# Linear attention and two expert layers on one core: routing in three rounds of 99 levels, GpSimd's order in the first expert, and one branch at the end

## The reference, cut to what matters

```python
state = alpha[:, :, t, :, None] * state + einsum(k[:, :, t], v[:, :, t])   # for each t
y[:, :, t] = einsum(q[:, :, t], state)
...
logits = x @ w_gate                       # 3072 x 8
for idx in np.argsort(-logits.flatten()): # greedy, the largest logit first
    tok, e = idx // E, idx % E
    if assigned[tok] >= 0 or counts[e] >= cap: continue
    assigned[tok] = e; counts[e] += 1
...
for e in range(E):
    out[assigned == e] = np.maximum(x[assigned == e] @ w1[e], 0.0) @ w2[e]
...
g = x @ w_gate2                           # x is the experts' output here
return (g / (1 + exp(-g)) * (x @ w_val)) @ w_out
```

## Time and profile before

| | |
|---|---|
| median of three runs | 913.92 us |
| the profiled execution | 914.68 us |
| its span in the profile | 912.9 us |
| PE busy | 853.5 us, 94% |
| VectorE busy | 512.2 us, 56% |
| ScalarE busy | 280.4 us, 31% |
| GpSimd busy | 253.2 us, 28% |
| mean granted TensorE clock | 0.966 |

### The profile page before, as it was taken

One profiled execution on the slowest core, in us unless ns is written; L12 is line 12 of the kernel. 1 busy time (PEld: TensorE's weight loads), 2 busy tenths in 40 slices (PEclk: granted clock), 3 DMA queues, 4 the chain that ended last, 5 costly groups with the idle time before them and its releaser, 6 DMA issues.

```text
span 912.9 us, 17432 instructions
## 1 busy us (share of the span) xinstructions
PE 853.5 (94%) x6582; PEld 801.4 (88%) x6582; DVE 512.2 (56%) x1057; ACT 280.4 (31%) x505; POOL 253.2 (28%) x200
## 2 busy tenths in 40 slices
PE   6999996699969999999999999999999999999991
PEld 4788874399869999999999999999999999999991
DVE  6999985637824464457445634664365536533330
ACT  1344441223214232422332332333233332333210
POOL 2322210165944023403240414050305130522001
PEclk8999997699979999999999999999999999999996
DMA  8789960400310022003200410030013002300000
GB/s 333 267 331 334 337 220 35 153 13 23 100 43 26 0 91 72 27 0 103 60 26 0 129 42 18 20 127 26 17 63 101 17 9 69 95 26 1 1 1 29
DMA packets 25858, 77.27 MB, mean 85 GB/s; under 512 B 3808, under 2 KB 10464, under 8 KB 22880
## 3 DMA queue, kind: packets, MB, share of 16 engines
q1 hardware_dynamic: 22752, 67.39, 21.2%
q0 software_dynamic: 3072, 9.44, 3.3%
HBM read 67.38 MB, written 9.44 MB: 84 GB/s over the span
## 4 chain that ended last, share of the span: by engine, by line
PE 74%; POOL 3%; DVE 2%; issue 1%; DMA 1%; ACT 0%; POOLq 0%; ACTq 0%
PE ps_up L1572 44%; PE ps_acc L1572 26%; PE ps_turn L818 2%; POOL gated_low L1231 2%; POOL w_low L1375 1%; PE ps_turn L1578 1%; PE ps_turn L838 0%; PE ps_turn L823 0%; DVE quick_at_row L794 0%; DMA x_tok<-x_rows,slot_token 0%; DMA x_tok<-x_rows,from_rows 0%; DVE quick_over_cut L740 0%; POOL out L1397 0%; PE ps_up L1578 0%; POOL x_tok L1369 0%
## 5 line engine op out<-in xcount | busy, mean ns | idle before, releaser
L1375 POOL TENSOR_TENSOR w_low<-w_raw,w_high 128x768 fp32r<-128x768 f32 x60 | 130.3, 2178 | 256.3 <-ACT w_high L1463 255.9
L1572 PE MATMUL ps_up<-z_high,gated_high 128*128 128x384 f32 x576 | 197.5, 343 | 0.2 <-DVE z_low L1530 0.2
L1572 PE MATMUL ps_up<-z_high,gated_low 128*128 128x384 f32 x576 | 195.7, 340 | 0.0
L1572 PE MATMUL ps_up<-z_low,gated_high 128*128 128x384 f32 x576 | 194.0, 337 | 0.0
L1572 PEld LDWEIGHTS ps_up<-z_high,gated_high 128*128 128x128 f32 x576 | 108.7, 189 | 0.9 <-issue 0.5
L1572 PEld LDWEIGHTS ps_up<-z_low,gated_high 128*128 128x128 f32 x576 | 108.7, 189 | 0.0
L1572 PEld LDWEIGHTS ps_up<-z_high,gated_low 128*128 128x128 f32 x576 | 108.6, 189 | 0.0
L1535 DVE TENSOR_TENSOR act_out<-ps_up,act_out 128x384 f32<-128x384 f32 x96 | 53.5, 558 | 94.5 <-ACT act_out L1479 92.7
L1482 ACT CAST u_high<-act_out 128x384 fp32r<-128x384 f32 x96 | 49.2, 513 | 170.5 <-DVE act_out L1539 170.5
L1572 PE MATMUL ps_acc<-gated_high,u_high 128*128 128x384 f32 x288 | 97.5, 339 | 1.8 <-DVE u_low L1542 1.8
L1572 PE MATMUL ps_acc<-gated_high,u_low 128*128 128x384 f32 x288 | 96.8, 336 | 0.0
(11 more groups left out here) (164 smaller groups left out, 1433.0 us busy)
## 6 DMA issues: line engine op xcount, KB each, us to landing
w_raw<-in_experts SPq DMA_DIRECT2D x64, 384.0 KB, 3.1
qka_in<-in_qka SPq DMA_DIRECT2D x23, 1026.0 KB, 8.4
gated_raw<-in_gated SPq DMA_DIRECT2D x12, 576.0 KB, 6.6
v_in<-in_v SPq DMA_DIRECT2D x24, 192.0 KB, 8.3
x_rows<-y_rows SPq DMA_DIRECT2D x24, 192.0 KB, 5.0
qka_in<-in_qka SPq DMA_DIRECT2D x1, 512.0 KB, 5.5
out<-o_tok,to_rows POOLq DMA_INDIRECT x24, 2.6
x_tok<-x_rows,from_rows POOLq DMA_INDIRECT x21, 3.2
```

What stands on the lines that cost most here:

```text
L1375: pool.tensor_tensor(w.low[:, m % RING, :], w.raw[:, m % RING, :], w.high[:, m % RING, :].bitcast(F32), ALU.subtract).then_inc(w_low_ready, 1)
L1572: mm = pe.matmul(acc, lhs[a], rhs[b], start=(first and i == 0), stop=(last and i == 2))
```

## The change

**Routing.** From the second phase on, three rounds of 99 levels (FINE_ROUNDS, FINE_CUTS = 100) take the place of four of 31; the first phase keeps its four rounds. The 24 count matmuls have 99 weight columns instead of 31. VectorE compares in two parts, tiles 0 to 14 at step 3n and tiles 15 to 23 at step 3n + 1, and writes into at_row instead of a buffer of its own; the count stands at step 3n + 1, the level matmul at step 3n + 2. The steps from the take on stay in the slots in which they were (STEPS_A_PHASE is 16). The choice of experts and the spread of levels stand at the last step of a phase, after the rows are listed. In the first phase they stand behind the parts of x that the first expert's products wait for (x_part). The levels of all three rounds are one table of 3 by 99, made from the numbers 1 to 99 and the range that is left.

**GpSimd.** w_low is written in two halves of 384 columns. In expert 0, w_low of the next expert's parts 0, 1, 2 stands behind gated_low 4, 5, 6 instead of 6, 7, 8; gated_low j waits (v_ready) for the products of gate_and_value(j - 4) instead of gate_and_value(j - 2), and for j below 4 for none; and the gather stands ahead of gated_low 10 and 11.

**The end.** The three blocks are one. Each engine has one branch, behind its last instruction of the layers; the exact routing and the second run of the layers are inside it, with the meetings (`meet`) that the blocks' barriers were. GpSimd always issues the last stores, and SyncE waits for them.

```diff
 ROUNDS = 4
+FINE_CUTS = 100
+FINE_ROUNDS = 3
+FINE_TILES = (slice(0, 15), slice(15, TILES))
...
+def has_failed(eng, quick):
+    eng.wait_ge(quick.judged, 1)
+    return eng.value_load(quick.failed[0:1, 0:1], min_val=0, max_val=1)
+def meet(eng, sem):
+    eng.drain().then_inc(sem, 1)
+    eng.wait_ge(sem, 5)
...
-    STEPS_A_PHASE = 2 * ROUNDS + 7
+    TAKE = 3 * FINE_ROUNDS
+    STEPS_A_PHASE = TAKE + 7
...
+    def rounds_before(self, p):
+        return FINE_ROUNDS * p + ROUNDS - FINE_ROUNDS
+    def compare(self, dve, tiles, cuts):
+        n = cuts.shape[-1]
+        tc = [P, tiles.stop - tiles.start, n]
+        dve.scalar_tensor_tensor(out=self.at_row[:, tiles, 0:n], in0=self.best[:, tiles].unsqueeze(2).broadcast_to(tc),
+                                 scalar=self.base[:, 0:1], in1=cuts.unsqueeze(1).broadcast_to(tc),
+                                 op0=ALU.subtract, op1=ALU.is_ge).then_inc(self.over_cut_ready, 1)
+    def find_full(self, dve, rounds, n):
+        dve.wait_ge(self.cuts_counted, rounds)
+        self.link(dve, dve.tensor_tensor(self.fills[0:n, :], self.ps_count[0:n, :], self.room_or_big[0:n, :], ALU.is_ge))
+        dve.tensor_reduce(self.cut_full[0:n, :], self.fills[0:n, :], AX_X, ALU.max).then_inc(self.cut_full_ready, 1)
+    def raise_base(self, dve, rounds, step):
+        dve.wait_ge(self.cut_found, rounds)
+        self.link(dve, dve.scalar_tensor_tensor(out=self.base[:], in0=self.ps_full, scalar=step, in1=self.base[:],
+                                                op0=ALU.mult, op1=ALU.add))
...
+        take = self.TAKE
+        n = s // 3
+        if s % 3 == 0 and 0 < s <= take:
+            self.raise_base(dve, self.rounds_before(p) + n, self.fine_cuts[:, n - 1, 0:1])
+        if s % 3 < 2 and s < take:
+            self.compare(dve, FINE_TILES[s % 3], self.fine_cuts[:, n, :])
+        if s % 3 == 2 and s < take:
+            self.find_full(dve, self.rounds_before(p) + n + 1, FINE_CUTS - 1)
+        if s == take:
+            self.take(dve)
+        if s == take + 1:
...
+        if s == take + 6:
+            self.choose(dve)
...
+    def choose(self, dve):
+        link = lambda ins: self.link(dve, ins)
+        te = [P, TILES, E]
+        open_cap = self.open_cap[:, :].unsqueeze(1).broadcast_to(te)
+        link(dve.tensor_tensor(self.limited[:], self.logits[:], open_cap, ALU.min))
+        link(dve.tensor_reduce(self.best[:], self.limited[:], AX_X, ALU.max))
+        link(dve.tensor_tensor(self.best[:], self.best[:], self.free_cap[:], ALU.min))
+        best = self.best[:, :].unsqueeze(2).broadcast_to(te)
+        link(dve.tensor_tensor(self.choice[:], self.limited[:], best, ALU.is_equal))
+        link(dve.tensor_tensor(self.width[:], self.high[:], self.low[:], ALU.subtract))
+        link(dve.tensor_scalar(self.fine_step[:], self.fine_scale[:], self.width[:, 0:1], None, ALU.mult))
+        fine = [P, FINE_ROUNDS, FINE_CUTS - 1]
+        link(dve.tensor_tensor(self.fine_cuts[:], self.numbers[:, 1:FINE_CUTS].unsqueeze(1).broadcast_to(fine),
+                               self.fine_step[:, :].unsqueeze(2).broadcast_to(fine), ALU.mult))
+        link(dve.tensor_copy(self.base[:], self.low[:]))
...
+        take = self.TAKE
+        n = s // 3
+        if s % 3 == 1 and s < take:
+            for i, tiles in enumerate(FINE_TILES):
+                pe.wait_ge(self.over_cut_ready, 2 * self.rounds_before(p) + 2 * n + i + 1)
                 for t in range(tiles.start, tiles.stop):
-                    mm = pe.matmul(self.ps_count[0:CUTS - 1, :], self.over_cut[:, t, :], self.choice[:, t, :],
-                                   start=(t == 0), stop=(t == TILES - 1))
+                    mm = pe.matmul(self.ps_count[0:FINE_CUTS - 1, :], self.at_row[:, t, 0:FINE_CUTS - 1],
+                                   self.choice[:, t, :], start=(t == 0), stop=(t == TILES - 1))
             mm.then_inc(self.cuts_counted, 1)
-        if s % 2 == 0 and 0 < s < last:
-            pe.wait_ge(self.cut_full_ready, ROUNDS * p + s // 2)
-            pe.matmul(self.ps_full, self.cut_full[:, 0:1].broadcast_to([CUTS - 1, P]), self.ones[0:CUTS - 1, 0:1],
-                      start=True, stop=True).then_inc(self.cut_found, 1)
-        if s == last:
+        if s % 3 == 2 and s < take:
+            pe.wait_ge(self.cut_full_ready, self.rounds_before(p) + n + 1)
+            pe.matmul(self.ps_full, self.cut_full[:, 0:1].broadcast_to([FINE_CUTS - 1, P]),
+                      self.ones[0:FINE_CUTS - 1, 0:1], start=True, stop=True).then_inc(self.cut_found, 1)
+        if s == take:
...
             def split_low(p, m):
                 pool.wait_ge(w_high_ready, FC * p + m + 1)
-                pool.tensor_tensor(w.low[:, m % RING, :], w.raw[:, m % RING, :],
-                                   w.high[:, m % RING, :].bitcast(F32), ALU.subtract).then_inc(w_low_ready, 1)
+                for n in range(2):
+                    cols = slice(n * DM, (n + 1) * DM)
+                    part = pool.tensor_tensor(w.low[:, m % RING, cols], w.raw[:, m % RING, cols],
+                                              w.high[:, m % RING, cols].bitcast(F32), ALU.subtract)
+                part.then_inc(w_low_ready, 1)
...
-                    for j in range(GC):
-                        if j >= 2:
-                            pool.wait_ge(v_ready, j - 1)
+                    for j in range(GC - 2):
+                        if j >= 4:
+                            pool.wait_ge(v_ready, j - 3)
                         w.split_gated_low(pool, j)
-                        if 6 <= j < 6 + RING - 1:
-                            split_low(e + 1, j - 6)
+                        if 4 <= j < 4 + RING - 1:
+                            split_low(e + 1, j - 4)
                 else:
                     for m in range(RING - 1):
                         split_low(e + 1, m)
                 pool.wait_ge(x_turned, K1 * e + K1)
                 gather(e + 1, 2 * e + 2)
+                if split_gated:
+                    for j in range(GC - 2, GC):
+                        w.split_gated_low(pool, j)
                 split_low(e + 1, RING - 1)
...
-                split_rest(E - 1)
-                if again:
-                    store(E - 1, 96 * (E - 1) + 48 - apart, 2 * E, one_by_one=False)
-                    pool.wait_ge(rows_moved, 96 * E - apart)
-                else:
-                    pool.wait_ge(quick.judged, 1)
-                    with pool.If(pool.value_load(failed[0:1, 0:1], min_val=0, max_val=1) < 1):
-                        store(E - 1, 96 * (E - 1) + 48 - apart, 2 * E, one_by_one=False)
-                        pool.wait_ge(rows_moved, 96 * E - apart)
-        @block.scalar
-        def _(act):
+            if again:
+                gather(0, 1)
+            else:
+                gather_first()
+            expert(0, split_gated=not again)
+            with pool.Fori(1, E - 1) as e:
+                expert(e)
+            split_rest(E - 1)
+            store(E - 1, 96 * (E - 1) + 48 - apart, 2 * E, one_by_one=False)
...
+            if not again:
+                quick.first_rounds_vector(dve)
+                quick.take(dve)
+                for s in range(quick.TAKE + 1, steps - 1):
+                    route(0, s, False)
+            for m in range(RING):
+                dve.wait_ge(w_high_ready, m + 1)
+                dve.tensor_tensor(w.low[:, m, :], w.raw[:, m, :], w.high[:, m, :].bitcast(F32),
+                                  ALU.subtract).then_inc(w_low_ready, 1)
+            for k in range(K1):
+                x_part(k, k, ps_acc[k])
+            if not again:
+                quick.choose(dve)
+                quick.end_first_phase()
+            with dve.Fori(0, E - 1) as e:
...
+        with nc.Block() as block:
+            @block.sync
+            def _(sp):
+                first.sync(sp)
+                with sp.If(has_failed(sp, quick) > 0):
+                    meet(sp, first_done)
+                    exact.sync(sp)
+                    meet(sp, exact_done)
+                    again.sync(sp)
```

464 lines of the change are left out of this document (224 added, 240 removed).

## The result

The changed kernel took 919.26 us (median of five runs, 917.88 to 921.45) against 913.92: a ratio of 1.0063, interval 1.0052 to 1.0074. I had predicted 911.5, with the time inside a range of 900 to 930 and "slower" at 0.29. The profiled execution took 919.26 too, span 917.4, so 4.6 us more than the profiled one of before.

What follows compares the result with a forecast made beforehand. PE, busy for 94% of the span, was taken as the bound. Terms -6.0 + 0.6 + 13.2 - 10.2 = -2.4 gave 912.3 us profiled, 911.5 against the 913.92 median; own range 905 to 919, wider range 900 to 930.

Steps and rivals of the forecast that it cites:

- rounds of 99 levels: Routing phases: three counts and level matmuls instead of four save 0.85 us a phase, seven times, -6.0 us.
- choice ahead of the first h_low: After the first phase, choosing experts stands between x_low and the first h_low, so PE waits: +0.6 us.
- periods of pieces 4, 5, 6: Expert 0: PE stands while POOL waits for w_high ahead of gated_low; periods of 12.4, 14.2 and 12.7 us.
- pieces 7 to 9: Expert 0 after the stands: three pieces of plain PE work, slow clock and the turn, 16.2 us.
- net of GpSimd's order: Expert 0, product of piece 4 to that of piece 10: 55.5 us instead of 42.3, +13.2.
- tail: Kernel's end: one branch under the copies and stores instead of flag loads and branches after POOL's drain, -10.2 us.
- a load in one pass: Count matmuls: reason given for 47 ns per 99-column weight load, bf16 being loaded in one pass as in the transposes.
- My bound of 56 ns a load: Count matmuls: upper end of the forecast's load pace of 41 to 56 ns, put at 3 us each way.
- A: Rival on count weight loads: 99 columns load as fast as 128, 10.2 us lower, 901.3 us; chance 0.12.
- B: Rival on count weight loads: slow streaming, 95 ns each, 24 us higher, 935.6 us; chance 0.15.
- C: Rival on expert 0: POOL never holds PE, 26.1 us below the forecast, 885.4 us; chance 0.08.
- the unknown 0.05: Whole kernel: chance of 0.05 left for outcomes covered by neither the forecast nor the named rivals.

Runs made afterwards that it cites:

- e7: Changed kernel with w_low back behind gated_low 6, 7, 8 and the gather behind the last gated_low: 898.33 us.
- e4: Changed kernel with fine_cuts made by three tensor_scalar instructions of one SBUF tensor each instead of one tensor_tensor of two: 921.12 us.
- e1: Changed kernel with w_low of the next expert's parts 0, 1, 2 back behind gated_low 6, 7, 8: 892.49 us.
- e2: Changed kernel with ScalarE's w_high of the next expert's parts one shared piece earlier: 903.82 us.
- e5: Kernel before with only the change's GpSimd order in expert 0 (w_low, v_ready wait, gather): 931.69 us.
- e6: Changed kernel with all twelve gated_low in a run without v_ready waits, then w_low 0 to 2, the gather, w_low 3: 895.74 us.
- e11: Kernel before without the exact routing and the second run of the layers: 904.73 us.

## Why the prediction was wrong

The prediction had the right mechanism in the place that mattered, and one term too small: 912.3 for the profiled execution, 919.3 measured.

| term, as predicted | predicted | measured |
|---|---|---|
| rounds of 99 levels | -6.0 | -3.8 (7 x 0.54) |
| choice ahead of the first h_low | +0.6 | +0.75 |
| periods of pieces 4, 5, 6 | 12.4, 14.2, 12.7 | 11.5, 13.5, 12.3 |
| pieces 7 to 9 | 16.2 | **25.7** |
| net of GpSimd's order | +13.2 | **+20.7** |
| tail | -10.2 | -11.1 |

**The step that failed** is "Pieces 7 to 9 then take 3 x 4.71 + 1.8 + 0.3 for the turn = 16.2". I had weighed what the gather's new place does to the gather, and to gated_low 10 behind it, and never asked what GpSimd's run behind the gather does to VectorE. My only line on their contention was GpSimd waiting for VectorE's at_row; the other direction was in the trace of before, where one u_low took 1.40 us, and at_row, the plainer sign, 3.41 instead of 1.75 beside w_low:

```profile
232.69 3.41 DVE L794 TENSOR_TENSOR quick_at_row<-quick_row,quick_row_numbers 128x1536 bf16<-128x1536 bf16 x1
```

Both are holds by one GpSimd instruction; no trace of before has one for a whole run. Of the 9.5 us missed, 5.5 are PE's wait for u_low. 1.65, 0.3 and 0.75 are the slow clock in the project, the turn and the product behind it. Another 1.2 is the slow clock after the third stand, which held for the whole product (6.12 us instead of 3.14, so 3.0 where I took 1.8). e7 shows the condition: with the gather behind the last gated_low there is no hold to the end of a run. e4 shows what it is not: a matter of two inputs. Without this stall of 8.2 us the profiled execution would have taken about 911, close to the 912.3 forecast, but partly by luck: the periods, the tail and the start came out 5.2 us better than I had them, and the rounds 2.2 worse.

**The rounds** were sized well link by link and too high in sum. The count took 1.10 + 0.14 = 1.24 (predicted 1.22), since 46 ns a load met the 47 that two rows gave. That was luck too: the same slope gives 15 ns for 31 columns, where the trace of before has 29, and nothing here tests the reason that I gave, a load in one pass. (My bound of 56 ns a load is worth 4.5 us over 504 loads, not the 3 that I wrote.) The level took 0.02 + 0.12 = 0.14 (predicted 0.11). That is 4.14 a phase against 3.99. The take's matmul L877 costs 0.04 more than L827 did. The remaining 0.1 of the 0.31 missing per expert lies in the plain products of 18 matmuls: five of the loop's expert take 3.16 us in the chain where their like took 3.13 to 3.15 before. Why, no run tells. The phase of expert 0 lies among its waits, so the 7 x 0.54 of the table is the loop's figure carried to it.

**The periods** came out as a chain of the links named, 2 us shorter in sum: in piece 4 w_low took 3.25 us instead of 2.19 but gated_low 2.88 instead of 3.28, so contention cost 0.7 where I had added 1.6. e1, e2 and e5 each turn one link and move the time by what the chain says. **The tail** is 0.9 better: GpSimd's drain ended 4.4 us after the last DMA instruction (912.7 to 917.1), and not 5.9 as before (897.15 to 903.0). **The start** was 2.3 us shorter for no edit that I priced. In the kernel after and in nine variants of it the first gather has landed at 174.5 to 174.9, and in the tenth, e6, at about 177.0; in the kernel before, e11 and e5 at 176.8, 175.6 and about 175.2. So the start can differ by over 2 us between kernels that have it alike, and how much of the 2.3 is the change's, no run tells.

**The rivals.** A (short loads) and B (long ones, by the column) both fell for 99 columns, as the 46 ns show; A's short load is real, but one must ask for 128 columns to have it, and it was 29 columns of nothing away. C (no stand, 885.4) could not come with ScalarE's order as it was; e1 comes near it from the other side, with w_low two pieces later. Of the 0.29 for "slower", 0.15 was B's. What came was my own forecast with one more stall of 8 us, and for that only 0.08 of the forecast and the unknown 0.05 stood.

## To carry to other kernels

When work moves on an in-order queue, follow what its input waits for: GpSimd's w_low moved two pieces ahead of ScalarE's w_high, and PE waited 17.7 us for what stood behind it, mended by two numbers. When a run of GpSimd instructions is put right behind a gather, look at what VectorE has to do in SBUF for the length of the whole run. And for small matmuls price the weight load by rows of the very shape, since a larger one can be the cheaper.
